# Attention and low-rank MLP block on one core: MLP steps placed between the score tiles of later batches, weights streamed per block, turned u kept in SBUF

## What is computed

```python
    q_rot, k_rot = (rotate(q), rotate(k))
    scale = 1.0 / np.sqrt(D)
    scores = scale * np.matmul(q_rot, k_rot.transpose(0, 1, 3, 2))
    scores = scores - np.max(scores, axis=-1, keepdims=True)
    attn = np.exp(scores)
    attn = attn / (np.sum(attn, axis=-1, keepdims=True) + 1e-09)
    return np.matmul(attn, v).astype(np.float32)
...
    xt = x.transpose(0, 2, 1)
    h = xt @ U @ V
    u = x + h.transpose(0, 2, 1)
    ch = np.maximum(u @ w_ch1, 0.0) @ w_ch2
    return (u + ch).astype(np.float32)
```

## Time and profile before

| | us |
|---|---|
| median of 3 runs (lowest, highest) | 798.92 (798.64, 800.2) |
| the profiled execution | 799.79 |
| its span, first to last instruction | 797.7 |
| busy: PE, PE's weight loads | 725.8, 655.4 |
| busy: ACT, DVE, POOL | 373.4, 373.0, 260.1 |
| mean granted clock of PE | 0.987 |

### The profile page before, as it was taken

One profiled execution on the slowest core, in us unless ns is written; L12 is line 12 of the kernel. 1 busy time (PEld: TensorE's weight loads), 2 busy tenths in 40 slices (PEclk: granted clock), 3 DMA queues, 4 the chain that ended last, 5 costly groups with the idle time before them and its releaser, 6 DMA issues.

```text
span 797.7 us, 11651 instructions
## 1 busy us (share of the span) xinstructions
PE 725.8 (91%) x4336; PEld 655.4 (82%) x4336; DVE 373.0 (47%) x619; ACT 373.4 (47%) x807; POOL 260.1 (33%) x182
## 2 busy tenths in 40 slices
PE   0799998989898989987499999999999999999998
PEld 0689887778787878775499999999999999999997
DVE  2689897788778897786411121121212112122112
ACT  1689998789878989774433211111210111111100
POOL 6667758556866658300455200000000000000000
PEclk9999999999999999999799999999999999999999
DMA  7856665577457753523763030011003003001001
GB/s 239 237 147 188 174 189 139 152 225 197 127 164 227 205 164 90 130 70 119 219 243 128 1 119 1 0 61 59 1 1 118 1 1 119 0 1 40 1 1 39
DMA packets 45942, 86.47 MB, mean 108 GB/s; under 512 B 7552, under 2 KB 20032, under 8 KB 43840
## 3 DMA queue, kind: packets, MB, share of 16 engines
q1 hardware_dynamic: 45456, 84.50, 35.9%
q10 hardware_dynamic: 432, 1.25, 0.4%
HBM read 43.25 MB, written 14.16 MB: 72 GB/s over the span
## 4 chain that ended last, share of the span: by engine, by line
PE 50%; DVE 1%; ACT 0%; issue 0%; DVEq 0%
PE ps L842 25%; PE ps L855 25%; DVE utl L802 1%; DVE res L809 0%; ACT wh L777 0%; DVE wl L813 0%; DVEq L808 0%
## 5 line engine op out<-in xcount | busy, mean ns | idle before, releaser
L819 DVE SCALAR_TENSOR_TENSOR htl<-ps,hth 128x384 fp32r<-128x384 f32 x96 | 53.5, 558 | 325.8 <-ACT hth L794 325.8
L794 ACT ACTIVATE hth<-ps 128x384 fp32r<-128x384 f32 x96 | 47.2, 492 | 328.1 <-PE ps L842 328.1
L496 DVE TENSOR_REDUCE negmax<-ps 128x1 f32<-128x576 f32 (+1 forms) x160 | 120.2, 751 | 55.1 <-PE ps L602 53.7
L602 PE MATMUL ps<-stack 128*128 128x288 f32 (+1 forms) x640 | 125.3, 319 | 22.3 <-DMA stack<-raw 22.3
L842 PE MATMUL ps<-uth,wh 128*128 128x384 f32 x384 | 130.1, 339 | 10.1 <-DVE utl L802 10.1
L412 ACT ACTIVATE prob<-ps,negmax 128x576 f32<-128x576 f32 (+1 forms) x160 | 118.4, 740 | 41.8 <-DVE negmax L496 40.9
L842 PE MATMUL ps<-uth,wl 128*128 128x384 f32 x384 | 130.0, 338 | 0.0
L842 PE MATMUL ps<-utl,wh 128*128 128x384 f32 x384 | 129.5, 337 | 0.0
L502 DVE TENSOR_TENSOR ptl<-ps,pth 128x512 fp32r<-128x512 f32 (+1 forms) x192 | 121.4, 646 | 3.6 <-ACT pth L421 1.9
L855 PE MATMUL ps<-wl,hth 128*128 128x512 f32 x288 | 114.0, 396 | 0.0
L620 PE MATMUL ps<-ident,prob 128*128 128x128 f32 (+1 forms) x672 | 97.7, 270 | 17.7 <-ACT prob L412 16.1
(11 more groups left out here) (65 smaller groups left out, 860.4 us busy)
## 6 DMA issues: line engine op xcount, KB each, us to landing
stack<-raw SPq DMA_DIRECT2D x192, 144.0 KB, 2.6
raw<-in_qk SPq DMA_DIRECT2D x16, 1152.0 KB, 5.5
tables<-in_w SPq DMA_DIRECT2D x11, 512.0 KB, 4.5
raw<-scratch_ut SPq DMA_DIRECT2D x6, 768.0 KB, 6.7
res<-scratch_u SPq DMA_DIRECT2D x18, 256.0 KB, 3.5
out<-res SPq DMA_DIRECT2D x18, 256.0 KB, 2.1
vraw<-in_v SPq DMA_DIRECT2D x16, 256.0 KB, 5.3
scratch_u<-xn SPq DMA_DIRECT2D x16, 256.0 KB, 3.2
```

The source lines that it names most:

```text
L496: nc.vector.tensor_reduce(negmax[0:w, n % NT:n % NT + 1], scores_of(n, w), AX.XY, ALU.max, negate=True).then_inc(maxed, 1)
L602: mm = nc.tensor.matmul(ps[0:w, at_:at_ + CH], stack[:, r % 2, i, 0, P * t:P * t + w], stack[:, r % 2, i, part, CH * c:CH * c + CH], start ...
L794: nc.scalar.activation(hth[:, i % 2], up_bank(i), ACT.Relu).then_inc(relu_hi, 1)
L819: nc.vector.scalar_tensor_tensor(htl[:, i % 2], up_bank(i), 0.0, hth[:, i % 2], ALU.max, ALU.subtract).then_inc(relu_lo, 1)
```

## The change

The two stages become one program of 177 slots. Slots 0 to 53 (`n < MERGED`) hold attention alone, much as before. From slot 54 on the scores have one pair of banks, the ring two banks, and the banks won go to `up` (one) and to the accumulators (one set of three). From slot 56 on a table of parts stands behind a slot's own work: a step of the MLP is cut into two halves of `up` and three tiles of `down`, in the order `up(i+1)`, `down(i)`, and `parts_by_slot` deals them out by written-in durations so that slots within a region end evenly. 77 parts stand in slots 56 to 92, 160 in 93 to 133, 60 in 134 to 159, 20 in 160 to 176, and 163 (33 steps) behind the last slot. A block of positions begins when the batches that it needs are turned.

The weights of each step are loaded anew for each of the 96 steps, three buffers deep, w1 and w2 apart (256 KB each), and split each time by ACT (L610, L614) and POOL (L495, L501): 192 roundings and 192 subtractions of 512 columns. Turned u is split straight out of PSUM into SBUF for two batches; u itself still goes to DRAM for the final addition. `pth`, `ptl` and the buffer of exponentials hold one head instead of more; the low part of the last 64 keys lies under its high part, so that `times_v` has 9 matmuls for 10. `low_rank` becomes five steps `low` of two matmuls, whose results DVE adds up in SBUF. The mix takes 13 slots for 33. At the start q and k of the first pair are rotated by DVE alone, k's half is loaded first, and ACT's queue issues part of the stacking DMAs.

```diff
+MERGED = 54
+PV_ALONE = {1: 0, 3: 1}
+PV_MERGED = {0: 0, 2: 1}
...
+MIX_MERGED = {3: [("natural", 0)], 4: [("natural", 1), ("low", 0)], 5: [("natural", 2), ("low", 1)],
+              6: [("natural", 3), ("low", 2)], 7: [("natural", 4), ("low", 3)], 8: [("low", 4)], 9: [("hidden", 0)],
+              10: [("residual", 0)], 11: [("residual", 1), ("turned_u", 0)], 12: [("residual", 2), ("turned_u", 1)],
+              13: [("residual", 3), ("turned_u", 2)], 14: [("residual", 4), ("turned_u", 3)], 15: [("turned_u", 4)]}
...
+PARTS = [("up", 0, 0), ("up", 0, 1)]
+for _i in range(STEPS):
+    if _i + 1 < STEPS:
+        PARTS += [("up", _i + 1, 0), ("up", _i + 1, 1)]
+    PARTS += [("down", _i, _t) for _t in range(TT)]
...
+REGIONS = ((MERGED + 2, 93, 77), (93, 134, 237), (134, NTILES, 297), (NTILES, SLOTS, 317))
...
+RING_ALONE, RING_MERGED = (4, 5, 6, 7), (6, 7)
+ACC, UP = (2, 3, 4), 5
...
+def parts_by_slot():
+    plan, done = {}, 0
+    for first, last, end in REGIONS:
+        goal = (sum(slot_ns(n) for n in range(first, last)) + sum(part_ns(x) for x in PARTS[done:end])) / (last - first)
+        spent = 0
+        for n in range(first, last):
+            spent += slot_ns(n)
+            start = done
+            while done < end and (n == last - 1 or spent + part_ns(PARTS[done]) / 2 < goal * (n - first + 1)):
+                spent += part_ns(PARTS[done])
+                done += 1
...
+            def load_w1(i):
+                if i >= WBUF:
+                    sp.wait_ge(up_done, i - WBUF + 1)
+                sp.dma_start(w1u[:, i % WBUF], w[i % FB][:, 0]).then_inc(w1_loaded[i % WBUF], 16)
+            def load_w2(i):
+                if i >= WBUF:
+                    _down_read(sp, i - WBUF, e)
+                sp.dma_start(w2u[:, i % WBUF], w[i % FB][:, 1]).then_inc(w2_loaded[i % WBUF], 16)
...
+                p, f = divmod(i, FB)
+                if kind == "up" and part == 1 and i + WBUF < STEPS:
+                    load_w1(i + WBUF)
+                if kind == "down" and part == TT - 1 and i + WBUF < STEPS:
+                    load_w2(i + WBUF)
...
+                for b, what, t in mixes_of(n - STORE_LAG):
+                    if what == "residual":
+                        store_u(b, t)
+                if n == PRIME - 3:
+                    for i in range(WBUF):
+                        load_w1(i)
+                        load_w2(i)
+                for x in MLP_AT.get(n, []):
+                    mlp(*x)
+            for x in MLP_REST:
+                mlp(*x)
...
+                                        ALU.subtract).then_inc(w1_lo, 1)
+            def w2_rest(i):
+                pool.wait_ge(w2_hi, i + 1)
+                at = i % WBUF
+                nc.gpsimd.tensor_tensor(w2l[:, at], w2u[:, at], w2h[:, at],
+                                        ALU.subtract).then_inc(w2_lo, 1)
+            def mlp(kind, i, part):
+                if kind == "up" and part == 1:
+                    if i + 2 < STEPS:
+                        w1_rest(i + 2)
+                    w2_rest(i)
...
+            prepare(1, ROPE_Q)
+            prepare(1, ROPE_K)
+            split_v(0)
...
+            def round_w1(i):
+                act.wait_ge(w1_loaded[i % WBUF], 16 * (i // WBUF + 1))
+                nc.scalar.activation(w1h[:, i % WBUF], w1u[:, i % WBUF], ACT.Copy).then_inc(w1_hi, 1)
+            def round_w2(i):
+                act.wait_ge(w2_loaded[i % WBUF], 16 * (i // WBUF + 1))
+                nc.scalar.activation(w2h[:, i % WBUF], w2u[:, i % WBUF], ACT.Copy).then_inc(w2_hi, 1)
...
+            def mlp(kind, i, part):
+                if kind == "up" and part == 1:
+                    act.wait_ge(up_done, i + 1)
+                    if i >= 2:
+                        _down_read(act, i - 2, e)
+                    nc.scalar.activation(hth[:, i % 2], up_bank(), ACT.Relu).then_inc(relu_hi, 1)
+                    if i + 2 < STEPS:
+                        round_w1(i + 2)
+                    round_w2(i)
...
+                if n >= MERGED:
+                    for unit in units[0:1]:
+                        round_p(*unit)
+                    if n < NTILES:
+                        exponentials(n)
+                    units = units[1:]
+                for unit in units:
                     round_p(*unit)
...
+            first_products(0)
+            first_lo(1)
+            first_sum(0)
+            first_lo(0)
...
+                if j in (TAIL, LAST):
+                    last = source.shape[1] - 1
+                    nc.vector.tensor_tensor(pth[D:P, NT - 1:NT, queries], source[0:D, last:last + 1],
+                                            pth[0:D, NT - 1:NT, queries], ALU.subtract).then_inc(pt_lo, 1)
...
+                    else:
+                        dve.wait_ge(h_sum, k)
+                        nc.vector.tensor_tensor(hsum[:, :], part, hsum[:, :], ALU.add).then_inc(h_sum, 1)
...
+                if kind == "up" and part == 1:
+                    dve.wait_ge(relu_hi, i + 1)
+                    nc.vector.scalar_tensor_tensor(htl[:, i % 2], up_bank(), 0.0, hth[:, i % 2],
+                                                   ALU.max, ALU.subtract).then_inc(relu_lo, 1)
...
+                if n >= MERGED:
+                    for unit in units_of(n - 1):
+                        split_p(*unit)
+                    for half in pv_of(n):
+                        add_halves(*half)
...
-                mine = products[NT:] if second else products[:NT]
-                for kt, part in mine:
-                    mm = nc.tensor.matmul(work(("pv", g, c), 0, P, CH), v2[:, (g // 2) % 2, kt, g % 2],
-                                          part[:, g % 2, kt, CH * c:CH * c + CH],
-                                          start=(kt, part) == products[0], stop=(kt, part) == products[-1])
...
-                if n >= SCORES:
-                    pe.wait_ge(expd, n - SCORES + 1)
+                    pe.wait_ge(stacked[g % HEADS_STACKED], STACKED * (g // HEADS_STACKED + 1))
+                if n > MERGED:
+                    pe.wait_ge(expd, n)
...
+                products = [(kt, part) for kt in range(NT - 1) for part in (pth, ptl)] + [(NT - 1, pth)]
...
+                pe.wait_ge(pt_lo, lows_done(g, LAST if c else TAIL))
...
+            def up(i, part):
+                p, f = divmod(i, FB)
+                if part == 0:
+                    pe.wait_ge(w1_lo, i + 1)
+                    if i == 0:
+                        _release(pe, left[UP], e)
+                    else:
+                        pe.wait_ge(relu_lo, i)
+                    if f == 0:
+                        pe.wait_ge(ut_lo, UT_NEEDED[p])
+                at = TB * (p % (UT // TB))
+                for d in range(2 * part, 2 * part + 2):
+                    hi, lo = uth[:, d, at:at + TB], utl[:, d, at:at + TB]
+                    for q, (l, r) in enumerate(((w1h, hi), (w1h, lo), (w1l, hi))):
+                        mm = nc.tensor.matmul(up_bank(), l[:, i % WBUF, P * d:P * d + P], r,
+                                              start=(d == 0 and q == 0), stop=(d == DB - 1 and q == 2))
+                if part == 1:
+                    mm.then_inc(up_done, 1)
...
+            def down(i, t):
+                p, f = divmod(i, FB)
+                if t == 0:
+                    pe.wait_ge(relu_lo, i + 1)
+                    pe.wait_ge(w2_lo, i + 1)
+                if f == 0:
+                    if p:
+                        pe.wait_ge(added, TT * (p - 1) + t + 1)
+                    elif ACC[t] < RING_ALONE[0]:
+                        pe.wait_ge(expd, MERGED)
+                    else:
...
+                for q, (l, r) in enumerate(((hth, w2h), (htl, w2h), (hth, w2l))):
+                    mm = nc.tensor.matmul(acc_bank(t), l[:, i % 2, P * t:P * t + P], r[:, i % WBUF],
+                                          start=(f == 0 and q == 0), stop=(f == FB - 1 and q == 2))
...
             for n in range(SLOTS):
                 if n < NTILES:
                     scores(n)
-                for second in (0, 1):
-                    if pv_of(n, second):
-                        times_v(*pv_of(n, second), second)
-                for unit in units_of(n - LAG):
+                if n < MERGED:
+                    for half in pv_of(n):
+                        times_v(*half)
+                for unit in units_of(n - 1):
                     transposes(*unit)
-                for item in mixes_of(n):
-                    if item[1] == "low_rank":
-                        low_rank(item[0])
-                    else:
+                if n < MERGED:
+                    for item in mixes_of(n):
                         mix(*item)
-def _phase_b(nc, ctx, e):
...
+                else:
+                    for half in pv_of(n):
+                        times_v(*half)
+                    for of, *x in sequence(n):
+                        if of == "mlp":
+                            mlp(*x)
+                        else:
```

(14 more changed lines are left out.)

1018 lines of the change are left out of this document (486 added, 532 removed).

## The result

The changed kernel takes **786.95 us** (median of 4 runs, 785.53 to 788.38), beside 799.56 (4 runs, 798.64 to 800.86) for the one before in the same session: a ratio of 0.984, 95% interval 0.981 to 0.987. The sign was right; the size was not, since 745 was forecast with a range of 722 to 774. Some 41 us of an expected gain of 54 are missing.

The account below looks back on a forecast made before the run. TensorE was taken to bound the kernel: full in the MLP, 70 us empty in attention and mixes. 126 to slot 54, 599 work, 15 waits and 3.5 end gave a 743.5 us span, 745 us median; range 722 to 774.

Parts of the forecast that it names:

- What bounds the kernel, the MLP and the weights: MLP stage: TensorE full at 4.19 us a step, 402 us in all; streamed weights hidden in the last 33 steps.
- Rival (c): Streamed weights decide: GpSimd's subtractions delay `down`, 30 us at 1.95 us each, gain gone from 2.3; chance 0.03 in full.
- 45 tiles at 1.755: Attention without MLP, slots 0 to 44: exponentials pace each tile at 1.755 us, 79 us in all.
- The mix of batch 0, 16.7 us with two thirds of them before slot 54, and slots 54 and 55: Slots 45 to 57: mix costs 16.7 us as before, 11 of it before slot 54, which TensorE reaches at 126.
- TensorE's work from slot 54 on, 7.9 a head: Slot 54 to the end: 21.2 heads 167 us, mixes 24 and 2.5, MLP 402, cut steps 3; sum 599.
- I had counted 298: Old kernel, 22.3 to 390.4 us: 32 heads and 4 mixes hold 298 of 368 us of TensorE, 70 empty.
- The prediction's estimate by that share, 320: Old kernel's same 368 us, judged by weight-load share: 87% full, 48 us empty where starts show 70.
- Rival (a): TensorE is fuller in attention than its starts say: 320 us for 298, 14 more from slot 54, 769; chance 0.10.
- Waits, 15 us in all: Merged slots: TensorE waits for score banks, the mix's `low` steps and batch 3's tail; 15 us, bounds 5 and 35.
- rival (b): Merged slots: five queues in fixed order wait 0.3 us more in each of 104 slots, 776 us; chance 0.09.
- Start: Start to first score tile: 17.5 us where it was 22.3, a gain of 5.
- some 2 for landing: Start: estimated time for the stacking DMAs to land before the first scores, some 2 us.

Follow-up runs that it names:

- experiment 10: Changed kernel plus a GpSimd copy of each down-weight block onto itself behind its subtraction; 798.46 us.
- Experiment 1: Changed kernel, first half of a head's products waiting for the tail strip's low part only before its last product; 778.67 us.
- experiment 2: Changed kernel, first half of a head's products put back one tile later, its wait left whole; 788.14 us.
- Experiments 5 and 9: First: changed kernel, batch 0's mix spread over slots 45 to 60, MLP parts five slots later, 791.09 us. Second: experiment 8's kernel, strips subtracted a slot sooner, 773.32 us.
- experiment 11: Edits of Experiment 1 and Experiment 6, two by two: plain 774.27; fillers 772.20; new order (mix behind next tile's scores) 766.51; new order and fillers 765.66 us.
- experiment 8: Edits of Experiment 1 and Experiment 6 together, plus 38 unread identity transposes (fillers) in front of three TensorE waits in slots 50, 52, 54; 771.20 us.
- Experiment 6: Changed kernel, 16 MLP parts moved from slots 134 to 159 into slots 160 to 176; 780.04 us.
- Experiment 4: Experiment 8's kernel, at the start head 1's stacks and the loads behind them issued only once head 0's stacks landed; 773.30 us.

## Why the prediction was wrong, step by step

**What bounds the kernel, the MLP and the weights: right.** The MLP stays 4.19 us a step, the last steps and the end take what was forecast to 0.5 us, no queue of weights decides, and GpSimd's low part comes 0.37 us early. Rival (c) didn't come, and its price was near: a spare of 0.4 us a step was forecast, and experiment 10 has 0.34 (0.61 less 0.27).

**Tiles 0 to 53, "45 tiles at 1.755": failed, 6.9 us.** The step took the pace of the old exponentials as if nothing on the path had moved. But the change puts a head's first products one tile sooner, folds the tail's low part into them and waits for it in full at their start; before, half of them started on three strips. I had costed the fold at a gain of one matmul and nothing for its wait. TensorE waits 6.6 us for it, in eight heads. Experiment 1 gives back 5.9 us up to slot 45 and 8.3 in all; by experiment 2 the first half in its old slot, with its wait whole, gives back 1.8.

**The mix of batch 0, 16.7 us with two thirds of them before slot 54, and slots 54 and 55: failed, 14.8 us, the largest piece.** The 16.7 came from a batch in which the mix had 33 slots. In 13 slots, nearly all without MLP parts around, each part goes through TensorE, VectorE, ScalarE and partly GpSimd in fixed queues, and TensorE's next tile stood behind it. Experiments 5 and 9 show that neither spacing nor sooner free banks help; experiment 11 that the order does, 7.8 us with the clock that follows it. Of 47.4 us in slots 45 to 55 the records have 10.3 us of idle time, and the clock was at its half level, 1.2 in place of 2.4 GHz, for some 20 us (0.85 of 34 and 0.62 of 13). The forecast had nothing for the clock. At a third of a us each (experiment 8) these 20 us are 6 to 7 us, an estimate. The clock fell at 132.0, 142.3 and 149.1 us, each within 1.5 us after the end of one of the waits shown above (1.54, 2.31, 2.14 us). That such waits bring it down fits this and experiments 6 and 11; which of them do, and when, isn't shown.

**TensorE's work from slot 54 on, 7.9 a head: 5 us too little.** For slots 56 to 159 the sum has 431 us of work. Measured are 444.0 less 8.0 of recorded idle time in front of matmuls, 436. In the kernel before, the same reading gives 368.1 less 45.9 of idle time, 322 us of work, which is what its busy column says (322.2) and I set aside; I had counted 298. I added up kinds of work, each timed by itself, and left out what lies between them. That this is all of the 24 us isn't shown: up to 5 are the half clock (three stretches of 3.4 us with matmuls in them). The Trainium skill ("Perfetto Trace Analysis", Identifying the Most-Contended Engine) says to judge TensorE's room by the busy share of its weight loads. The prediction's estimate by that share, 320, agrees with the 322, and my count doesn't. Rival (a) thus had the better figure for the kernel before; forward it asked for 14 us more and 5 came.

**Waits, 15 us in all.** In slots 56 to 159 8.0 us against 6: right, and rival (b) is out (the scores wait 1.3 us for exponentials, three times). In the tail 7.2 against 6, with a half clock that I hadn't priced; those slots took 7.0 over forecast. Experiment 6 took 6.9 off the kernel's time, some 4.8 of it there.

**Start: failed, 4.0 us.** The failed term is "some 2 for landing". With two issues it made 3.4 us from ScalarE's first stacking DMA to the first scores. In the changed kernel that is 7.8:
```profile
13.67 3.26 ACTq L321 DMA_DIRECT2D stack<-raw  x4
...
21.48 1.30 PE L842 MATMUL ps<-stack 128*128 128x288 f32 x4 [21.48 <-DMA stack<-raw]
```
In experiment 4, with one head's stacks on the way, it is 4.0 (14.04 to 18.05). It had the first scores 2.7 us sooner than the kernel that it was made on, and showed that this wasn't worth having by itself.

**What stays open.** 765.7 is still 21 over the forecast. Slots 45 to 59 take 54.3 us in the best kernel against the plan's 37.2, heads 9.3 to 9.4 against 8.8. What paces a head then wasn't tried; the 0.84 us that ScalarE waits in slot 41 while VectorE takes two low parts before the row maximum are a candidate.

## What to carry to other kernels

When work is folded together, ask of each wait which of the instructions behind it really needs it, and put it there: one operand that comes late held nine matmuls in each of eight heads. A helper's steps between tiles are priced by their chain over the engines and by what each in-order queue holds behind them, not by their busy time; let the engine issue the next tile's work before it waits for the helper's data. And check a count by kinds against the whole stretch (length less recorded idle time) before adding it up for a stretch that doesn't exist yet: here that check was at hand, in the busy column, and would have shown 24 us. Last, before crediting an edit with a difference of a few us, compare the granted clocks: two executions of one kernel, with the same instructions and different granted clocks, differed by 3.3 us in one stretch.

## What the runs showed of the hardware

The stretches with waits of 0.7 to 2.3 us between short bursts of matmuls ran in part at a granted clock of half (products 0.24 apart, not 0.13), and how much of them differed between executions of one kernel: 7 and 18 us of slots 45 to 59, for 59.4 and 62.7 us (experiment 8). With the plain kernel of experiment 11 four runs had mean clocks from 0.987 to 0.996 and times from 776.65 to 770.88, and the one with new order and fillers 0.998 to 1.000 and a spread of 0.9 us. Transfers from SBUF to SBUF of two heads' stacks at once moved some 200 GB/s and took 6 to 7 us from issue to landing (medians 6.0 and 6.9), against a median of 2.7 before, where one queue issued them 0.6 us apart. GpSimd's copy of a 128x512 tile took 0.61 us, its subtraction 1.29.
